# A banded attention and two gated networks on one core: chunk by chunk through both networks, with the following chunk's attention spread beside both

## What is computed

```python
def reference(q, k, v, n_sink, window, moe_*, moe2_*):
    # attention: 2 x 8 heads, 768 positions, 64 features; each position sees itself,
    # the 127 before it, and the first 4 positions ("sinks")
    scores = q @ k.T / 8;  scores[not (is_sink | in_window)] = -1e9
    a = exp(scores - max) / (sum + 1e-9);  x = (a @ v) as 1536 tokens x 512
    # first network, 512 -> 2048 -> 512
    h = x @ w_in;   x = (h * sigmoid(1.702 * h)) @ w_out
    # second network, 512 -> 1536 -> 512
    out = (sigmoid(x @ w_gate) * (x @ w_val)) @ w_out2
```

## Time and profile before

| | us |
|---|---|
| median of 3 runs | 742.49 |
| the three runs | 741.49, 742.49, 3560.62 |
| span of the profiled execution | 739.4 |
| TensorE busy | 694.5 (94%) |
| VectorE busy | 383.3 (52%) |
| ScalarE busy | 313.8 (42%) |
| GpSimd busy | 321.3 (43%) |

### The profile page before, as it was taken

One profiled execution on the slowest core, in us unless ns is written; L12 is line 12 of the kernel. 1 busy time (PEld: TensorE's weight loads), 2 busy tenths in 40 slices (PEclk: granted clock), 3 DMA queues, 4 the chain that ended last, 5 costly groups with the idle time before them and its releaser, 6 DMA issues.

```text
span 739.4 us, 11003 instructions
## 1 busy us (share of the span) xinstructions
PE 694.5 (94%) x3632; PEld 570.3 (77%) x3632; DVE 383.3 (52%) x1056; ACT 313.8 (42%) x644; POOL 321.3 (43%) x167
## 2 busy tenths in 40 slices
PE   7777799899999889999999999999999999999998
PEld 5566588777787778778888887888888888888886
DVE  6897668868777785887433234211241122312212
ACT  4787356536655664655432243222232222322311
POOL 2573324454553545442443463344434433443330
PEclk9999989999999999999999999999999999999999
DMA  7322513243314223302223332322242223423001
GB/s 207 117 72 85 170 57 114 83 137 103 112 57 157 85 72 115 125 33 75 97 86 111 131 129 86 124 88 86 92 179 86 85 102 111 142 87 111 17 0 58
DMA packets 24299, 73.63 MB, mean 100 GB/s; under 512 B 3968, under 2 KB 3968, under 8 KB 24256
## 3 DMA queue, kind: packets, MB, share of 16 engines
q1 hardware_dynamic: 24256, 73.09, 29.5%
HBM read 69.93 MB, written 3.15 MB: 99 GB/s over the span
## 4 chain that ended last, share of the span: by engine, by line
PE 70%; DVE 10%; issue 4%; ACT 4%; DVEq 0%; POOL 0%; ACTq 0%
PE ps L890 17%; PE ps L892 17%; PE ps L891 17%; PE ps L935 4%; PE ps L936 4%; PE ps L937 4%; DVE probs_sink L666 3%; DVE probs_n L668 2%; ACT w_hi L494 1%; ACT pt_hi L506 1%; PE ps L842 1%; PE ps L861 1%; DVE g_hi L734 1%; PE ps L862 1%; DVE x_lo L781 1%
## 5 line engine op out<-in xcount | busy, mean ns | idle before, releaser
L433 POOL TENSOR_TENSOR w_lo<-w_raw,w_hi 128x1024 fp32r<-128x1024 f32 (+1 forms) x84 | 242.8, 2890 | 287.8 <-ACT w_hi L494 287.3
L890 PE MATMUL ps<-x_hi,w_hi 128*128 128x512 f32 (+1 forms) x480 | 189.4, 394 | 0.4 <-DVE x_lo L679 0.3
L892 PE MATMUL ps<-x_hi,w_lo 128*128 128x512 f32 (+1 forms) x480 | 187.7, 391 | 0.0
L891 PE MATMUL ps<-x_lo,w_hi 128*128 128x512 f32 (+1 forms) x480 | 187.4, 390 | 0.0
L494 ACT ACTIVATE w_hi<-w_raw 128x1024 fp32r<-128x1024 f32 (+1 forms) x84 | 104.1, 1240 | 110.5 <-PE ps L937 66.0
L746 DVE TENSOR_TENSOR gated<-ps,squashed 128x512 f32<-128x512 f32 x36 | 24.9, 691 | 212.5 <-ACT squashed L562 212.5
L892 PEld LDWEIGHTS ps<-x_hi,w_lo 128*128 128x128 f32 x480 | 90.4, 188 | 19.3
L890 PEld LDWEIGHTS ps<-x_hi,w_hi 128*128 128x128 f32 x480 | 90.4, 188 | 19.2 <-DVE x_lo L679 0.8
L891 PEld LDWEIGHTS ps<-x_lo,w_hi 128*128 128x128 f32 x480 | 90.5, 189 | 17.8
L562 ACT ACTIVATE squashed<-ps 128x512 f32<-128x512 f32 x36 | 21.5, 598 | 144.6 <-PE ps L892 144.6
L890 PE MATMUL ps<-g_hi,w_hi 128*128 128x512 f32 x192 | 78.0, 406 | 0.0
(11 more groups left out here) (82 smaller groups left out, 1092.1 us busy)
## 6 DMA issues: line engine op xcount, KB each, us to landing
w_raw<-in_w SPq DMA_DIRECT2D x36, 768.0 KB, 4.3
w_raw<-in_w SPq DMA_DIRECT2D x48, 512.0 KB, 3.3
q_raw<-in_q_t SPq DMA_DIRECT2D x48, 128.0 KB, 3.0
k_raw<-in_k_t SPq DMA_DIRECT2D x48, 128.0 KB, 3.0
v_raw<-in_v_t SPq DMA_DIRECT2D x12, 256.0 KB, 2.8
out_x<-out_sb SPq DMA_DIRECT2D x12, 256.0 KB, 2.7
v_sink_raw<-in_v_sink SPq DMA_DIRECT2D x4, 160.0 KB, 2.6
k_sink_raw<-in_k_sink SPq DMA_DIRECT2D x8, 8.0 KB, 2.5
```

Of the source, the lines that this page charges most:

```text
L433: pool.tensor_tensor(w_lo[:, slot, 0:n], w_raw[:, slot, 0:n], w_hi[:, slot, 0:n].bitcast(F32), ALU.subtract).then_inc(w_ready, 1)
L890: pe.matmul(ps[:, bank, :], hi, act_hi, start=first, stop=False, skip_group_check=True)
L891: pe.matmul(ps[:, bank, :], hi, act_lo, start=False, stop=False, skip_group_check=True)
L892: return pe.matmul(ps[:, bank, :], lo, act_hi, start=False, stop=last, skip_group_check=True)
```

## The change

- **Order of the work.** A chunk passes through the first network (16 steps) and right on through the second (12 steps) before the next chunk begins. A chunk is 28 steps or 272 quanta.
- **The attention of the following chunk** (32 units) is spread beside both networks of a chunk: one slot every 8 quanta for the first 15, then one every 7 3/8 (`slot_base`). A slot's parts no longer stand together: score at offset 0, normalise at 2, the transposes of the unit before at 3, its `transposed_high` and `pt_low` at 4, its `weigh` at 6, the copy of four units' sum at 7.
- **Banks.** Scores and transposes of the late units take turns in one bank. The bank that comes free doubles the hidden bank of the first network; in the second, gate and value have one bank each instead of two. `squashed` has two buffers.
- **Unrolled.** No loop is left. The early attention keeps its order. The sinks' parts are split twice in all, at the start and once between units of the attention; the copied mask is gone. The accumulators are no longer set to zero but started by their first matmul.
- The sigmoid of the second network is made by Tanh with scale 0.5 and a later factor of one half.

The core of the diff, in this order: tables of positions, banks, the list of ScalarE, the attention's parts and the list of VectorE, then score, transposes, hidden blocks and the list of TensorE.

```diff
-QUANTA = 2 * KT
-LATE_W_LAG = 3
-SLOT_AT = {n * 27 // 10 + 2: n for n in range(UNITS + LATE_W_LAG)}
-EARLY_WEIGHTS = (11, 15, 19)
...
+CHUNK_UNITS = CH // P * H
+ALL_UNITS = TILES * H
+LAST_UP = F1 - 1
+def quanta_of(c, r):
+    if r == LAST_UP:
+        return 3 * KT
+    if r < LAST_UP:
+        return 2 * KT
+    if r < PER_CHUNK - 1:
+        return 3 * KT
+    return 2 * KT if c < NCH - 1 else KT
+def first_quantum(c, r):
+    return sum(quanta_of(c, i) for i in range(r))
+HOLE = 15
+OFF_SCORE, OFF_NORMALISE, OFF_TRANSPOSE, OFF_WEIGH = 0, 2, 3, 6
+OFF_SPLIT, OFF_PT, OFF_X = 1, 4, 7
+def slot_base(n):
+    return 8 * n if n < HOLE else 127 + (n - HOLE) * 59 // 8
+def parts_at(c, q):
+    if c == NCH - 1:
+        return []
+    return [(off, n) for n in range(CHUNK_UNITS + 1) for off in range(8) if slot_base(n) + off == q]
...
-        H_BANK = 0
+        H_BANKS = [0, 5]
+        GATE_BANK, VALUE_BANK = H_BANKS
         Y_BANKS = [1, 2, 3, 4]
-        S_BANK, T_BANK, O_BANK = 5, 6, 7
-        early = Flow(2 * UNITS, 2, 3, 4, 5, 3, [S_BANK, H_BANK], [T_BANK, 1], [O_BANK, 2], fillers=2)
-        late = Flow(UNITS, 1, 2, 2, LATE_W_LAG, 2, [S_BANK], [T_BANK], [O_BANK], fillers=0)
+        ST_BANK, O_BANK = 6, 7
...
-        GATE_BANKS, VALUE_BANKS = [0, 5], [6, 7]
+        def s_bank(u):
+            return early.s_banks[u % 2] if u < CHUNK_UNITS else ST_BANK
+        def t_bank(u):
+            return early.t_banks[u % 2] if u < CHUNK_UNITS else ST_BANK
+        def o_bank(g):
+            return early.o_banks[g % 2] if g < CHUNK_UNITS // GROUP else O_BANK
...
+                for r in range(PER_CHUNK):
+                    step = PER_CHUNK * c + r
+                    for j in range(quanta_of(c, r)):
+                        if j == 0 and step + AHEAD < STEPS:
+                            weights_high(step + AHEAD)
+                        if r == LAST_UP and 1 <= j <= KT:
+                            y_high(c, j - 1)
+                        if j == (2 * KT if r == LAST_UP else KT):
+                            squash(step + 1)
+                        if r == PER_CHUNK - 1 and j == quanta_of(c, r) - 1:
+                            copy_even(c, 0)
+                        attention_at(c, first_quantum(c, r) + j)
+                copy_even(c, 2)
...
+            def attention_at(c, q):
+                for off, n in parts_at(c, q):
+                    u = CHUNK_UNITS * (c + 1) + n
+                    if off == OFF_SCORE and n < CHUNK_UNITS:
+                        dve.wait_ge(scored, u + 1)
+                        mask_and_max(u)
+                    if off == OFF_NORMALISE and n < CHUNK_UNITS:
+                        guard(u)
+                        invert(u)
+                        normalise(u)
+                        if u + 1 == TPS * H:
+                            k_sinks(1)
+                    if off == OFF_PT and n > 0:
+                        pt_low(u - 1)
+                    if off == OFF_X and n > 0 and (u - 1) % GROUP == GROUP - 1:
+                        x_low((u - 1) // GROUP)
+                        if u == TPS * H:
...
+                for r in range(PER_CHUNK):
+                    step = PER_CHUNK * c + r
+                    for j in range(quanta_of(c, r)):
+                        if r == LAST_UP and 2 <= j <= KT + 1:
+                            y_low(c, j - 2)
+                        if r < LAST_UP or (r == PER_CHUNK - 1 and c < NCH - 1):
+                            if j == KT + 1:
+                                gate(step + 1)
+                                split_gated(step + 1)
+                        elif LAST_UP < r < PER_CHUNK - 1:
+                            if j == 2 * KT:
+                                gate(step + 1)
+                                split_gated(step + 1)
+                        if r == PER_CHUNK - 1 and j == quanta_of(c, r) - 1:
+                            copy_odd(c, 1)
+                        attention_at(c, first_quantum(c, r) + j)
+                    if r == LAST_UP:
+                        gate(step + 1)
+                        split_gated(step + 1)
...
+            def score(u):
+                h, bank = u % H, s_bank(u)
+                if u % GROUP == 0:
+                    pe.wait_ge(qk_low, 2 * (u // GROUP + 1))
+                if u == TPS * H:
+                    pe.wait_ge(k_sinks_ready, 2)
+                if u < CHUNK_UNITS:
+                    wait_from(pe, masked, u - 1)
+                else:
+                    pe.wait_ge(masked, u)
+                    pe.wait_ge(pt_ready, u - 1)
+                pe.matmul(ps[:, bank, 0:KC], q_hl[:, h, :], k_hi[:, h, :], start=True, stop=False)
                 pe.matmul(ps[:, bank, 0:KC], q_hl[:, h, :], k_lo[:, h, :], start=False, stop=True).then_inc(scored, 1)
...
+            def transpose(u):
+                bank, g = t_bank(u), u // GROUP
                 pe.wait_ge(normalised, u + 1)
-                wait_count(pe, pt_ready, u + 1 - banks, least + n + 1 - banks)
-                if n % GROUP == GROUP - 1:
-                    pe.transpose(ps[0:GROUP * NS, bank, 2 * P:3 * P], probs_sink[:, n // GROUP % 2, :], ident[:, :])
-                pe.transpose(ps[:, bank, 0:P], probs_n[:, n % flow.buffers, 0:P], ident[:, :])
-                pe.transpose(ps[:, bank, P:2 * P], probs_n[:, n % flow.buffers, P:2 * P], ident[:, :]).then_inc(transposed, 1)
...
+            def hidden(step, k):
+                c, r = divmod(step, PER_CHUNK)
+                if k == 0:
+                    pe.wait_ge(w_ready, step + 1)
+                    wait_from(pe, gate_done, step if r == 0 else step - 1)
+                    if r == 0:
+                        pe.wait_ge(x_ready, 2 * 8 * (c + 1) - 2)
+                if k == KT // 2 and r == 0:
+                    pe.wait_ge(x_ready, 2 * 8 * (c + 1))
+                last = from_x(H_BANKS[r % 2], step, 0, k)
+                if k == KT - 1:
+                    last.then_inc(hidden_done, 1)
+            def gate(step, k):
+                c, r = divmod(step, PER_CHUNK)
+                if k == 0:
+                    pe.wait_ge(w_ready, step + 1)
+                    pe.wait_ge(gate_done, step - 1)
+                    pe.wait_ge(squash_done, step)
+                if r == F1:
+                    pe.wait_ge(y_ready, KT * c + k + 1)
+                last = from_x(GATE_BANK, step, 0, k)
+                if k == KT - 1:
+                    last.then_inc(gate_summed, 1)
+            def value(step, k):
+                if k == 0:
+                    pe.wait_ge(gate_done, step)
+                last = from_x(VALUE_BANK, step, DM, k)
+                if k == KT - 1:
+                    last.then_inc(hidden_done, 1)
...
+            def attention_at(c, q):
+                for off, n in parts_at(c, q):
+                    u = CHUNK_UNITS * (c + 1) + n
+                    if off == OFF_SCORE and n < CHUNK_UNITS:
+                        score(u)
+                    if off == OFF_TRANSPOSE and n > 0:
+                        transpose(u - 1)
+                    if off == OFF_WEIGH and n > 0:
+                        weigh(u - 1)
...
+                for r in range(PER_CHUNK):
+                    step = PER_CHUNK * c + r
+                    for j in range(quanta_of(c, r)):
+                        attention_at(c, first_quantum(c, r) + j)
+                        k, part = j % KT, j // KT
+                        if r < LAST_UP:
+                            hidden(step + 1, k) if part == 0 else down1(step, k)
+                        elif r == LAST_UP:
+                            down1(step, k) if part == 0 else gate(step + 1, k) if part == 1 else value(step + 1, k)
+                        elif r < PER_CHUNK - 1:
+                            gate(step + 1, k) if part == 0 else value(step + 1, k) if part == 1 else down2(step, k)
+                        elif c < NCH - 1:
+                            hidden(step + 1, k) if part == 0 else down2(step, k)
```

More of the change, by code:

```diff
@@ L37 @@
 TILES = B * TPS
-PAIRS = TILES // 2
-UNITS = 2 * H
 GROUP = 4
@@ L347, in _ @@
-            with sp.Fori(0, 2) as i:
-                beside(0, i)
-            for c in range(1, NCH):
-                for i in range(2):
-                    beside(c, i)
-            def second(c, i, last):
-                for j in range(4):
-                    step = STEPS1 + F2 * c + 4 * i + j
-                    ahead = 4 * i + j + LOADED
-                    if not last or step + LOADED < STEPS:
-                        load_weights2(step + LOADED, (j + LOADED) % RING, ahead if j + LOADED < 8 and not last else ahead % F2)
@@ L460, in _ @@
[L460 to L469 removed]
+                    weights_low(EARLY_WEIGHTS.index(n))
@@ L858, in weigh @@
                 for slot in range(2):
                     values_hi, values_lo = v_hl[:, slot, h, 0:D], v_hl[:, slot, h, D:2 * D]
-                    high, low = (pt[:, n % 2, slot * P:slot * P + P] for pt in (pt_hi, pt_lo))
```

(36 more changed lines are left out.)

800 lines of the change are left out of this document (312 added, 488 removed).

## The result

| | before | after |
|---|---|---|
| median, us | 741.99 | 768.61 |
| span of the profiled execution, us | 739.4 | 767.7 |
| ratio of the times | | 1.0355, 95% interval 1.033 to 1.038 |

One of the four executions of each kernel was far slower (3560.6 and 986.7 us); the ratio leaves these out, and the other three of the changed kernel took 767.3 to 769.5 us.

What follows compares the result with a forecast made beforehand. TensorE, busy 94% of the span, was taken as the bound. Span 739.4 less 33.8 waste is 705.6; plus 20.4 (first network), 24 (second) and 1 (turns) gives 751.0, so 754 us, range 731 to 768.

Steps and rivals of the forecast that it cites:

- the second network: Waits of TensorE beside the second network of chunks 0 and 1: 13.8 us a chunk, 27.6 in two, taken as 24.
- The units' own time: TensorE's time for 64 late attention units when nothing waits: 0.88 us each plus 0.10 for sinks, 62.7 us.
- The first network: Waits in front of `weigh` beside the first network of chunks 0 and 1: 10.2 us a chunk, 20.4 in two.
- GpSimd holds VectorE longer: Rival: `normalise` or `g_hi` also waits for GpSimd's `k_lo`, `q_hl`, `v_hl`; 770 span, 766 as its middle; chance 0.22.
- Turns and clock: Turns between networks: nothing to 0.9 us each where one `down1` covers squash, gate and split; 1 us for three.
- The clock falling in the waits I hold unlikely: TensorE's clock was held unlikely to fall to its lower level in its waits; no time was added for it.
- Unrolling at 0: Removing the loops: a loop's turn costs TensorE nothing that can be seen, so 0 us.
- Removed waste: TensorE's waits for attention, the sinks' split and the low clock behind it: 33.8 us off 739.4, if all hidden.
- Hidden after all: Rival: tanh, gate and weights never fall on the short chain, 10 us of waits left; 719 us; chance 0.08.
- as many waits as before: Rival: the new order keeps about 27 us of waits for the same 64 units; 736 us; chance 0.20.
- `probs_sink`: Sign in the trace after: `probs_sink` of up to 3.5 us in the second network.

Runs made afterwards that it cites:

- `pt_hi` in front: Changed kernel with `pt_hi` in front of the squash of the same quantum in ScalarE's list, not behind it: 763.2 us, ratio to before 1.026.
- the pieces: Changed kernel with GpSimd's `w_lo` in pieces of 256 columns (4 or 6 instructions instead of one): 750.8 us, ratio to before 1.011.
- all three edits: Changed kernel with `weigh` a slot later, `pt_hi` in front of the squash and `w_lo` in pieces of 256 columns: 722.5 us, ratio to before 0.972.
- the lag: Changed kernel with `weigh` one slot later, 7 quanta instead of 3 behind the transposes (6 or 7 in places): 733.6 us, ratio to before 0.987.

## Why the prediction was off in size

The direction and the chain that was too short were right. Two terms of the sum were too small: the second network (24, measured 30.0) and what lies outside the attention's groups (1, measured 8.2). Point by point, in the spans: forecast 751, measured 767.7.

- **The units' own time** was forecast 62.7, for either order. The shortest groups of each kind add up to 62.1 in both traces (a plain unit takes 0.87 in a row, and 0.24, 0.23 and 0.41 in parts). What standing alone costs lies behind the groups: the next few products start 0.235 instead of 0.227 apart. That is 2.0 us before, behind 76 groups, and 4.6 after, behind 192. The sum took the 2.0 away as waste and added nothing.
- **The first network,** 0.3 us behind each squash and over 1 us with sinks: right in kind; in size 0.3 (plain), 1.3 to 1.6 (sinks, forecast 1.1), 2.0 and 1.4 in slots 13 and 14 of chunk 0 and 2.0 and 0.6 in chunk 1 (forecast 1.65 each). Two chunks: 22.2 against 20.4.
- **The second network.** The forecast's table gave 27.6, and the sum took 24, "some of these stand on a tenth of a microsecond". Measured 30.0. This rounding down had no row behind it. The table itself was too high in front of `weigh` (23.3 measured) and too low in front of the transposes: it let the mask be late in slots at j = 8 alone, by 0.35 us, and the transposes lost 5.9 us at four places. It let the gate and its split take 1.9 us always, but `g_hi` and `g_lo` are held by GpSimd just as `normalise` is. In slot 16, the first whose score lies in the second network (j = 2), `g_hi` took 3.44 us:

```profile
206.77 3.51 POOL L372 TENSOR_TENSOR w_lo<-w_raw,w_hi 128x1536 fp32r<-128x1536 f32 x1 [4.46 <-ACT w_hi L421]
207.13 3.44 DVE L591 CAST g_hi<-gated 128x512 fp32r<-128x512 f32 x1
...
211.21 0.42 DVE L540 CUSTOM_DVE_ANT_0 scores<-ps,masks 128x260 f32<-128x260 f32 x1
...
211.78 0.27 PE L715 MATMUL ps<-ident,probs_sink 128*16 128x128 f32 x1 [1.37 <-DVE neg_max L540]
```

  The mask stands behind it and the transposes wait for the mask, 1.4 us where the forecast had none. In slot 25 (j = 8) they wait 1.1 us at 274.3, because two copies for `x_lo` (0.86 us) stand in front of the mask beside the gate and its split. The rival "GpSimd holds VectorE longer" named the hold of `g_hi` and gave 766; its mechanism is what the trace shows, at fewer places than it counted.
- **Turns and clock** were forecast 1 us, measured 8.2 outside the groups: 1.6 at the turns of the networks (0.96 of it a `down1` that waits for `g_lo` at 663 us), about 1.8 in products at the lower clock behind waits of 2.1 and 1.8 us (and about 1 more inside the groups), and the 4.6 of the first point. "The clock falling in the waits I hold unlikely" was wrong: the earlier trace rows show waits of before that left it alone, but it fell behind two of the longest. Why behind these two and not behind the 1.84 us wait at 187 us stays open. The runs of the experiments don't settle it: it fell behind waits of 1.82 and 2.08 us with `pt_hi` in front, and not behind one of 2.08 with the pieces or one of 2.22 with all three edits.
- **The early attention,** whose list is unchanged, took 2.3 us longer. The windows of 30 to 60 us, with the same columns, before and then after:

```profile
30.00:60.00 30.00, 23.76 (x200) 18.09 (x199) 28.19 (x114) 24.69 (x71) 18.00 (x13) 1.00 0.29 88
```

```profile
30.00:60.00 30.00, 24.14 (x185) 19.24 (x184) 26.58 (x109) 22.59 (x65) 18.07 (x13) 0.89 0.24 68
```

  The unrolled kernel before, whose early part is that of before, shows it as well:

```profile
30.00:60.00 30.00, 24.09 (x187) 19.29 (x186) 26.77 (x108) 22.56 (x65) 17.95 (x13) 0.90 0.24 69
```

  In the nine profiles of this case the early part ends between 86.9 and 92.0 us. So this is the granted clock of an execution, not the change, and one profile can't carry such a difference.
- The sum: waits of the attention 52.1 against 44.4, turns, clock and the products behind groups 8.2 against 1, the early part 2.3, the units' own time 0.6 less: 16.6 of the 16.7 us between the spans. In the time it is 14.6: the forecast added 3.1 us to its span, while a timed execution lies some 1.8 us above its own span, and the profiled one (769.5) was 0.9 slower than the median.
- **Unrolling at 0** was right, by the run of its own. **Removed waste** was right in part: the wait for the sinks and the low clock behind it are gone, at 89.5 us the matmuls go on without a gap. The 2.0 us behind the groups were not removed.
- **"Hidden after all" (719) and "as many waits as before" (736)** were wrong for this order, but the lag shows that the second was near: with three or four quanta more in the chain the same kernel is at 733.6.
- **`probs_sink`** was forecast at up to 3.5 us in the second network; the longest took 2.75.

## What to carry over

When a unit of side work is cut into parts and spread out, compare for each part the room in the schedule with its own chain *plus the longest instruction that can stand in front on each engine it passes through*; the busy shares don't show it, and one quantum of room was worth 30 us here. An instruction of GpSimd that runs for 2.4 to 3.5 us should be cut into pieces when VectorE's casts and scalings lie on a short chain beside it. Count waits from the start-to-start distances of TensorE's matmuls: the list of waits missed a third of them.

## What the runs showed of the hardware

- A VectorE `tensor_scalar` over 4 columns took 214 to 2745 ns, depending on the GpSimd instruction that ran beside it; with the `w_lo` work in pieces of 256 columns, at most 881. The same showed for a cast from SBUF to SBUF (`g_hi`, 0.43 us, up to 3.45) and for a subtraction with both inputs in SBUF (`g_lo`, 0.69 us, up to 1.67), and not for those that read PSUM (`pt_lo`, at most 0.43).
- The cut made GpSimd busy for some 50 us more (320 to 372), and that cost nothing that could be seen in the time: 12 us were gained in the kernel before, 18 in the changed one.
- TensorE ran at the lower level of its clock behind one wait of 2.1 us and one of 1.8 us and not behind others as long; in the early part the low stretches lie at different places in kernels with the same list (granted clock of 30 to 60 us: 1.00, 0.89 and 0.90 in three profiles).
- Behind a group of the attention's matmuls the next few products started 0.235 instead of 0.227 us apart, where nothing waited.
